# Five column rounds of 480, 480, 480, 480 and 384 in place of 512, 512, 512, 384 and 384, with the default DMA scratch

## The reference

```python
p_packed = sm_attn(p, k, v)                 # 8 batches, 8 heads, 32 packs, 64 dims
out = sm_attn(q, p_packed, p_packed)        # 576 tokens of each batch
x = out.transpose(0, 2, 1, 3).reshape(4608, 512)

xn = x / sqrt(mean(x * x) + 1e-6) * rms_g
x = (silu(xn @ w_gate) * (xn @ w_val)) @ moe_w_out       # d_ff 1536

h = x @ w_in                                             # 512 -> 2048
g = maximum(h, 0) + alpha * minimum(h, 0)
out = g @ moe2_w_out                                     # 2048 -> 512
```

## Time and profile before

| | |
|---|---|
| time, median of 3 runs | 1434.79 us (1434.64 to 1435.7) |
| the profiled execution: time, span | 1434.79 us, 1433.0 us |
| PE busy | 1421.2 us (99%) |
| DVE, ACT, POOL busy | 959.9, 715.7, 318.5 us |
| second stage on PE | from 737.9 us to the end |
| granted TensorE clock | full in all 40 slices |

### The profile page before, as it was taken

The page is one execution under the profiler, slowest core; times in us unless marked ns, Lnnn a source line. Parts: engine busy times, 40 slices in busy tenths (PEclk is TensorE's granted clock), DMA queues, the critical chain, the costliest instruction groups (busy, mean ns, idle before and its releaser), DMA issues.

```text
span 1433.0 us, 24192 instructions
## 1 busy us (share of the span) xinstructions
PE 1421.2 (99%) x9334; PEld 1220.2 (85%) x9334; DVE 959.9 (67%) x1530; ACT 715.7 (50%) x1174; POOL 318.5 (22%) x543
## 2 busy tenths in 40 slices
PE   8999999999999999999999999999999999999998
PEld 4988878888887878879888888888888889999998
DVE  6775756647565575752337887688857886886786
ACT  4455454445544544442235664556545653664564
POOL 2803545244453423541910000000000000000000
PEclk9999999999999999999999999999999999999999
DMA  9414586876868687257227677758775868798775
GB/s 358 145 42 136 161 285 184 240 220 174 270 157 276 181 231 236 88 171 242 98 81 253 232 263 229 272 198 304 221 258 187 281 204 293 274 330 280 255 264 188
DMA packets 173747, 313.93 MB, mean 219 GB/s; under 512 B 22209, under 2 KB 118977, under 8 KB 159169
## 3 DMA queue, kind: packets, MB, share of 16 engines
q1 hardware_dynamic: 173488, 312.33, 66.7%
q10 hardware_dynamic: 144, 0.07, 0.0%
HBM read 250.10 MB, written 54.92 MB: 213 GB/s over the span
## 4 chain that ended last, share of the span: by engine, by line
PE 95%; DVE 2%; DMA 2%; ACT 1%; issue 1%; SPq 0%; DVEq 0%; ACTq 0%
PE psum L924 30%; PE psum L926 29%; PE psum L925 29%; PE psum L1122 3%; DMA rest_mid<-act_sb 1%; PE psum L1023 1%; PE psum L947 1%; PE psum L996 1%; DMA k_sb<-k_t 0%; DVE g_sb L1990 0%; DMA a_keys<-a_mid 0%; PE psum L1052 0%; PE psum L1051 0%; PE psum L1055 0%; ACT below L1572 0%
## 5 line engine op out<-in xcount | busy, mean ns | idle before, releaser
L924 PE MATMUL psum<-an_hi,m_hi 128*128 128x288 f32 x768 | 232.2, 302 | 1.4 <-DVE an_lo L1830 1.2
L925 PE MATMUL psum<-an_hi,m_lo 128*128 128x288 f32 x768 | 225.9, 294 | 0.0
L926 PE MATMUL psum<-an_lo,m_hi 128*128 128x288 f32 x768 | 225.7, 294 | 0.0
L924 PE MATMUL psum<-stage_hi,ring 128*128 128x512 f32 (+1 forms) x560 | 205.9, 368 | 0.3
L926 PE MATMUL psum<-stage_lo,ring 128*128 128x512 f32 (+1 forms) x560 | 205.6, 367 | 0.0
L925 PE MATMUL psum<-stage_hi,ring 128*128 128x512 f32 (+1 forms) x560 | 205.5, 367 | 0.0
L926 PE MATMUL psum<-x_lo,ring 128*128 128x512 f32 (+1 forms) x560 | 205.5, 367 | 0.0
L924 PE MATMUL psum<-x_hi,ring 128*128 128x512 f32 (+1 forms) x560 | 205.5, 367 | 0.0
L925 PE MATMUL psum<-x_hi,ring 128*128 128x512 f32 (+1 forms) x560 | 205.5, 367 | 0.0
L1562 ACT CAST stage_hi<-g_sb 128x512 fp32r<-128x512 f32 (+1 forms) x240 | 137.8, 578 | 117.3 <-PE psum L926 117.2
L924 PE MATMUL psum<-h_hi,ow_hi 128*128 128x512 f32 (+2 forms) x480 | 183.0, 381 | 0.1
(11 more groups left out here) (183 smaller groups left out, 2448.8 us busy)
## 6 DMA issues: line engine op xcount, KB each, us to landing
ring<-w_down SPq DMA_DIRECT2D x70, 1024.0 KB, 5.2
ring<-w_up SPq DMA_DIRECT2D x40, 1024.0 KB, 5.2
gv_sb<-w_gv SPq DMA_DIRECT2D x39, 1024.0 KB, 5.8
ring<-w_up SPq DMA_DIRECT2D x40, 768.0 KB, 4.4
k_sb<-k_t SPq DMA_DIRECT2D x16, 576.0 KB, 5.2
q_sb<-q_t SPq DMA_DIRECT2D x8, 1152.0 KB, 5.5
w_up<-parts_hi SPq DMA_DIRECT2D x16, 448.0 KB, 6.4
w_up<-parts_lo SPq DMA_DIRECT2D x16, 448.0 KB, 6.1
```

Of the source, the lines that this page charges most:

```text
L924: nc.tensor.matmul(dst, w_hi, hi, start=start, stop=False, skip_group_check=onto)
L925: nc.tensor.matmul(dst, w_lo, hi, start=False, stop=False, skip_group_check=onto)
L926: return nc.tensor.matmul(dst, w_hi, lo, start=False, stop=stop, skip_group_check=onto)
```

## The change

The widths of the five rounds become 480, 480, 480, 480 and 384 (the sum stays 2304), so the rounds take 960 tokens four times and 768 once, and `STARTS` follows. `WMAX` becomes 480, `WPAD` stays 512. The scratch that is kept free at the start of SBUF for DMA descriptors goes from 8192 bytes of each partition to the default, 16384, so all tiles move up by 8192 bytes; the tiles with `WMAX` columns shrink.

```diff
-WIDTHS = [512, 512, 512, 384, 384]
+WIDTHS = [480, 480, 480, 480, 384]
 STARTS = [2 * sum(WIDTHS[:t]) for t in range(len(WIDTHS))]
 ROUNDS = len(WIDTHS)
 assert 2 * sum(WIDTHS) == TOKENS
...
-    nc = bacc.Bacc("TRN2", target_bir_lowering=False, num_devices=1, dynamic_dma_scratch_size=8192)
+    nc = bacc.Bacc("TRN2", target_bir_lowering=False, num_devices=1)
```

## The result

The changed kernel is slower, by half a per cent. Its median is 1443.06 us over 5 runs (1441.87 to 1444.24) against 1435.06 us (1434.64 to 1435.7), a ratio of 1.0054 with a 95% interval of 1.004 to 1.0069. The time lies inside the wide range of 1430.4 to 1444 us, but outside the forecast's own 1434 to 1436 us, and the difference is clear of the noise. The forecast of no change did not come true; what came true is the rival "a matmul of 480 columns does not settle", to which I had given a chance of 0.20 and the time 1443 us.

The account below looks back on a forecast made before the run. TensorE's own stream was taken as the bound; matmuls, stall, DMAs and tail each added 0, so the 1433.0 us span plus 1.8 us around it gave 1434.8 us. Own range 1434 to 1436 us, wider 1430.4 to 1444 us.

Parts of the forecast that it names:

- a matmul of 480 columns does not settle: Rival, chance 0.20: in all halves of rounds 0 to 3, 1.6 to 5.0 ns more each; +8 us, 1443 us.
- What bounds the kernel: Whole kernel: TensorE's own stream decides, PE busy 1421.2 of 1433.0 us; DVE and ACT not near the bound.
- The matmul at 480: Rounds 0 to 3: 2688 matmuls at 213.3 ns take 573.4 us, the same as before; difference nothing.
- The bound from above: Matmuls of rounds 0 to 3: if 480 never settled, up to 5.0 ns more each, 13.4 us.
- the break-even of 1.07 ns: Matmuls of rounds 0 to 3: distance off the line, 2.6 cycles each, at which the result stops being "same".
- The third estimate: Matmul of 480 columns on a line drawn from 288 through 384: 214.9 ns, +4.4 us.
- The stall at unit 6: PE's wait for that unit's split in down halves: 0.88 us before, 0.89 us after; no difference.
- DVE and ACT: Second stage: they need 655 and 594 ns per PE unit of 1.28 us, so they stay covered.
- The DMAs: Weight loads, x pieces and stores: paced by TensorE, cost 0; half the x pieces 7% slower by rule.
- The first stage, the scratch, the addresses: Before round 0 and in SBUF layout: 1 us less GpSimd work hidden, larger scratch and 8192-byte move worth nothing.
- the prediction's own sign: Profile after: forecast wrong if the first stage ends elsewhere than at 737.9 us.
- The chances: Odds for the whole kernel's time: same 0.55, slower 0.28, faster 0.17.

Follow-up runs that it names:

- the streams alone: Separate kernel of 96-matmul streams, one width each, nothing beside them, in several orders and byte shifts; unshifted, 480 columns took 216.7 ns a matmul, 512 took 226.7.
- the lead-in run: Changed kernel with its 480 columns begun 128 bytes later, plus 48 extra matmuls of 480 columns before round 0; median 1457.52 us, profiled execution 1454.33 us.

## Why the prediction came out as it did, step by step

- **What bounds the kernel**: right. PE has no idle time in the wide halves, before and after, and the whole difference is the distance between starts.
- **The matmul at 480**: this is the step that failed. "On the line through rows 3 and 4 it costs 213.3 ns"; it costs 216.7 ns, and 2688 x 3.33 = 9.0 us. The mistake was to take two equal points for a law: 512 and 384 lie on a line of slope one clock per column because both are at a floor of 32 cycles, and between them the overhead rises to 40. The bound from above held (it allowed 5 ns), and the break-even of 1.07 ns was sound. The third estimate that I worked out and did not take, the line through 288 and 384, gave 214.9 ns, on the right side but only half of the way: the 288-wide row was a sign that the overhead is not constant, and I set it aside as "outside and far shorter".
- **The rival's mechanism**: its size was right (3 ns, 1443 us), its reason was not, and that the two meet is in part luck. I had it that 480 might never come to a steady distance; in truth it settles at once, on a pattern with a higher mean. The 5.0 ns of the earlier trace rows, from which the price was taken, are something else, a start that passes. Twelve distances on, the same stream of 512 columns is back at its 226 to 227 ns and stays there, here eight distances in 1.81 us:

```profile
702.54 0.39 PE L924 MATMUL psum<-h_hi,ow_hi 128*128 128x512 f32 x1
...
704.35 0.39 PE L926 MATMUL psum<-h_lo,ow_hi 128*128 128x512 f32 x1
```

That what went before can matter for good, no row of the kernel before showed; the streams alone and the lead-in run do.
- **The stall at unit 6**: predicted 0.12 us in each of four rounds and 0.41 us in the last; measured no wait in the four, and in the last round one of 0.5 us at the weight load, as before (0.46 us). The split was forecast ready at 7.69 us, and at 216.7 ns its matmul is due 0.12 us later than at 213.3: the slower stream hid its own wait, and the four terms of 0.12 us fell away. The term itself was sound. In the lead-in run the stream did have 213.3 ns up to unit 6, and there the weight load waited until 826.97 - 819.29 = 7.68 us.
- **DVE and ACT**: L2002 and L1562 take 654 and 594 ns at 480 columns, as forecast (655 and 594).

```profile
L2002 DVE TENSOR_TENSOR stage_lo<-g_sb,stage_hi 128x480 fp32r<-128x480 f32 x192 | 123.8, 654 | 37.8 <-ACT stage_hi L1562 37.7
```

- **The DMAs**: right that they cost nothing. A piece of x of 480 KB takes as long as one of 512 KB did (7.4 us), the DMA share of the down half of round 3 fell from 0.92 to 0.78, and ACT's wait at L1599 is gone. By the rule of the Trainium skill, "DMA: Bandwidth & Descriptors", "How a descriptor splits into AXI transactions", half of such pieces would be 7% slower for their size, an estimate: a row of 1920 bytes that begins 128 bytes behind a 256-byte boundary would take the time of one of 2048. Equal medians for 480 and 512 KB are no proof against that. The packets are: in each of the four first loads of x, two of which begin at a second column block, 208 to 248 of 256 packets of 1920 bytes took 79 ns, and in the kernel before the most frequent time for 2048 bytes was 84 ns. No extra time for the displaced rows shows.

```profile
x_raw<-y_mid SPq DMA_DIRECT2D x13, 480.0 KB, 7.4
```

- **The first stage, the scratch, the addresses**: right at nothing, shown by the run with the widths alone. By the prediction's own sign, a first stage that ends elsewhere than at 737.9 us, it would have been wrong, for it ended at 736.75 us. That sign was too narrow: with the first stage untouched the second began at 737.67 us in the run with the widths alone and at 739.89 us in the one with 496 columns. Moving all tiles together by 192 bytes did nothing either, in the run with shifted columns; what costs is a new distance between columns and weights (64 and 128 bytes: 1447.0 and 1445.5 us against 1443.1).
- **The chances**: "same" at 0.55 was too much for a sum whose only open term had no row at its width and a break-even of 1.07 ns. Of the bounds for that term, 211.7 to 218.3 ns, 3.9 ns lay above what counts as "same" (213.3 + 1.07 ns) and 0.6 ns below it, and the chances should have followed them.

Open remains what inside TensorE makes these patterns, and why of two waits of 0.17 and 0.16 us at 448 columns only the second changed the pattern. That they come of how the reading of columns and the loading of weights fall together is argued from the shifts (moving the weights alone changes the price at 512), not shown.

## What to carry to other kernels

Where TensorE is busy without a gap, its price for a matmul of a width that the kernel doesn't yet use has to be measured in the kernel's own pattern before widths are changed: 8 cycles on each of 2688 matmuls were half a per cent of this kernel. Equal sums of columns are not equal times, and two widths on one line don't vouch for the widths between them. A width whose best price can be lost at a short wait, as at 496 and 448 here, should be reckoned at its price after the wait.

## What the hardware showed that I had not expected

- A float32r matmul with its own weight load cost its columns and 32 cycles at best (28 at 288), and up to 48 cycles at 448 and 480 (206.7 and 220.0 ns) and 50 at 512 (234.3 ns), by place and history. At 224 columns it is 111.7 ns at every place.
- A shift of 128 bytes, of columns or of weights, cost a stream of 512 columns 6.7 ns a matmul, 3%.
- The same instructions at the same addresses ran at 213.4 or 217.8 ns a matmul for a whole half round, by what had run ahead of them; a single wait of 0.16 to 0.24 us changed the distance for all matmuls of that width that followed, from 202.7 to 206.7, from 220.0 to 223.3 and from 213.3 to 217.8 ns. Another wait of 0.17 us, at 448 columns, changed nothing.
